# Joining attention and the first dense layer of a three-part kernel into one block

## The chip, the cores and the metric

The kernel runs on one core of a Trainium2 chip. The metric is device time in microseconds (us) of one execution. Five engines of the core matter: TensorE (PE: matmuls and transposes; PEld are its weight loads), VectorE (DVE), ScalarE (ACT), GpSimd (POOL) and SyncE (SP, which here only issues transfers). Each runs its own list of instructions in order, and the lists wait for one another through semaphores.

## The reference

Everything is float32. Attention with a memory term for 4 batches of 8 heads, 576 tokens, 64 columns a head:

```python
scores = where(causal, -1e9, q @ k.T / sqrt(64))
local = softmax(scores) @ v
q_p = where(q > 0, q, exp(q) - 1) + 1
mem_out = (q_p @ M_prev) / (q_p @ z_prev + 1e-6)
x = g * mem_out + (1 - g) * local          # g = sigmoid(beta), heads side by side: 2304 x 512
```

Two dense layers follow:

```python
h = x @ w_in                               # 2304 x 2048
x = (s * maximum(h, 0) ** 2 + b) @ w_out   # 2304 x 512
h = x @ w2_in                              # 2304 x 1024
out = layernorm(h * softmax(h)) * g_ln @ w2_out
```

## The kernel before

There are three parts, each in a Block of its own: attention, the first layer, the second layer. At the end of a Block all engines meet at a barrier. The tensors of a part lie in SBUF and PSUM memory that the next part uses again. What passes from part to part is xT, the tokens turned so that features lie on partitions (4 blocks of 128 features by 2304 tokens), and the small staging buffer of class Stage for raw weights.

**Attention** goes over 32 heads in steps h = -6 to 34; heads come in 16 pairs. Each engine has its own program over the same steps, and at step h the PE works on three heads: scores of head h + 2 (first_rows, second_rows, third_rows, whose row maxima DVE takes from PSUM), the transposed scores of head h (cross, four chunks, of which ACT takes the exponentials in exp_weights and POOL masks the diagonal tiles in mask_weights, L345), and the weighing of the values of head h - 1 (weigh_values, L493, 30 small matmuls, which wait for all masks of that head). After a pair, DVE scales the result (scale_local, L703 to L711), POOL adds the memory half (add_halves, L352, 128x640), the PE turns it (turn_output, L388, five transposes) and ACT copies it into xT (copy_output, L583). The last pair, number 15, does this in steps 32 to 34. The first 512 tokens of xT, all that the first chunk of the layer needs, come from pairs 0 to 3 and are long done by then. SP loads queries, keys and values ahead, and at step 28 the first two blocks of both weight matrices of the layer into the staging buffer (load_win, load_wout).

**The first layer** takes the tokens in five chunks (512, 512, 512, 384, 384), and 16 blocks f of 128 hidden features. A float32 product is made of three rounded ones: a value is cut into a rounded part (hi) and the rest (lo), and hi*hi, lo*hi, hi*lo are summed. For chunk 0, ACT rounds four token blocks (x_hi, L900) and DVE subtracts (x_lo, L903). POOL cuts the weights: for each f first the w_in block (L823 rounds, L826 subtracts, 128x512 each), then the w_out block (L829, L832). The PE then runs hidden(c, f), 12 matmuls into ps_h (L857 to L859), and two blocks later output(c, f), 12 matmuls into ps_y (L872 to L874). Between them stand ACT's relu (L919), DVE's square and scale (L952, L954), ACT's rounding (L925) and DVE's subtraction (L957, g_lo). Inside hidden and output of chunk 0 the waits for weights are

```python
if c == 0:
    pe.wait_ge(win_cut, f + 1)
...
if first:
    pe.wait_ge(wout_cut, f + 1)
pe.wait_ge(g_lo_done, c * FT + f + 1)
```

SP loads w_in block f when block f - 2 is cut (its staging place is then free), and the same for w_out.

**The second layer** goes over 18 tiles of 128 tokens, with a barrier ahead of it in both kernels.

Of the kernel before, what the change touches and what calls it, by code (L numbers as in the profile page):

```python
# [6 lines left out]
F32 = mybir.dt.float32  # L7
# [5 lines left out]
P = 128  # L13
# [14 lines left out]
class Stage:  # L28
# [7 lines left out]
    def __init__(self, nc, ctx, w_in, w_out, v_in, v_out, g_ln):  # L36
        self.w_in, self.w_out, self.v_in, self.v_out, self.g_ln = w_in, w_out, v_in, v_out, g_ln
        self.rows = ctx.enter_context(nc.sbuf_tensor("stage", [P, 4, self.SLOT], F32))
        self.ln_gain = ctx.enter_context(nc.sbuf_tensor("ln_gain", [P, g_ln.shape[0] // P], F32))
# [42 lines left out]
def attention(nc, ctx, xT, q, k, v, M_prev, z_prev, beta, stage):  # L82
# [32 lines left out]
    def sem(name):  # L115
        return ctx.enter_context(nc.semaphore(name))

    q_raw = [sb(f"q_raw{s}", [P, NT, 2, D]) for s in range(2)]
    k_raw = [sb(f"k_raw{s}", [P, NT, 2, D]) for s in range(2)]
    v_raw = [sb(f"v_raw{s}", [P, NT, 2, E1]) for s in range(3)]  # L120
    mz = sb("mz", [P, NPAIR, 2 * E1])
    qT = [sb(f"qT{s}", [P, S]) for s in range(2)]
    cut = [sb(f"cut{s}", [P, 3, S], F32R) for s in range(2)]
    relu_q = [sb(f"relu_q{s}", [P, S]) for s in range(2)]
    fT = [sb(f"fT{s}", [P, W]) for s in range(2)]
    stacked = sb("stacked", [P, 2 * SLOTS, 2, W], F32R)
    Q1, K1 = sb("Q1", [P, SLOTS, 2, W], F32R), sb("K1", [P, LATE, 2, W], F32R)
    least = [sb(f"least{s}", [P, P]) for s in range(2)]
    negT = sb("negT", [P, P])
    pT = [sb(f"pT{s}", [P, NP]) for s in range(2)]  # L130
    spent = sb("spent", [P, sum(keys)])
    rm, rl = sb("rm", [P, NT, 2]), sb("rl", [P, 2, NT])
    t_mem = [sb(f"t_mem{s}", [P, NT, 2, D]) for s in range(3)]
    t_loc = sb("t_loc", [P, NT, 2, D])
    xq = sb("xq", [P, NT, 2 * D])
    mask = sb("mask", [P, FULL * P + P])
    ident = sb("ident", [P, P])
# [46 lines left out]
    STEPS = range(-6, HEADS + 3)  # L184
# [10 lines left out]

    block = ctx.enter_context(nc.Block())
# [17 lines left out]
    @block.sync  # L214
    def _(sp):
# [50 lines left out]
        for h in range(HEADS + 3):  # L266
# [16 lines left out]
    @block.gpsimd  # L283
    def _(pool):
# [70 lines left out]

        for h in STEPS:
            pr = h // 2
            even = h % 2 == 0
            if is_head(h):
                mask_weights(h, 0)  # L360
            if is_head(h + 1):
                if is_head(h):
                    pool.wait_ge(tri_done, h * NT + 2)
                else:
                    pool.wait_ge(phi_done, 1)
                spread_maxima(h + 1)
            if even and is_pair(pr + 2):
                round_queries(pr + 2)
            if is_head(h):
                mask_weights(h, 1)  # L370
            if even and is_pair(pr + 2):
                cut_queries(pr + 2)
            if h == -2:
                clear_keys()
            if not even and is_pair(pr - 1):
                add_halves(pr - 1)
            if is_head(h):
                mask_weights(h, 3)
            if even and is_pair(pr + 1):
                features(pr + 1)  # L380

    @block.tensor
    def _(pe):
# [114 lines left out]

        for h in STEPS:
            pr, even = h // 2, h % 2 == 0  # L500
            ahead, here, behind = is_head(h + 2), is_head(h), is_head(h - 1)
            if ahead or is_head(h + 1):
                first_rows(h + 2)
            if here:
                cross(h, 0)
            if even and is_pair(pr - 2):
                turn_output(pr - 2)
            if h == 0:
                memory(0)
            if not even and is_pair(pr + 3):  # L510
                turn_queries(pr + 3)
            if behind:
                weigh_values(h - 1, (0, 1))
            if ahead:
                second_rows(h + 2)
            if here:
                cross(h, 1)
            if behind:
                weigh_values(h - 1, (2,))
            if even and is_pair(pr + 3):  # L520
                turn_keys(pr + 3)
            if ahead:
                third_rows(h + 2)
            if here:
                cross(h, 2)
            if behind:
                weigh_values(h - 1, (3,))
            if here:
                cross(h, 3)
            if not even and is_pair(pr + 1) and pr + 1 > 0:  # L530
                memory(pr + 1)
            if behind:
                weigh_values(h - 1, (4,))

    @block.scalar
    def _(act):
# [57 lines left out]
        for h in range(-2, HEADS + 3):  # L594
            pr, even = h // 2, h % 2 == 0
            here = is_head(h)
            if here:
                exp_weights(h, 0)
            if even and is_pair(pr - 2):
                copy_output(pr - 2)  # L600
            if not even and is_pair(pr + 3):
                copy_queries(pr + 3)
            if here:
                exp_weights(h, 1)
            if is_pair(pr + 2):
                if even:
                    repeat_queries(pr + 2, 0)
                else:
                    feature_relu(pr + 2)
            if even and is_pair(pr + 3):  # L610
                round_keys(pr + 3)
            if here:
                exp_weights(h, 2)
            if is_pair(pr + 2):
                if even:
                    repeat_queries(pr + 2, 1)
                else:
                    feature_exp(pr + 2)
            if here:
                exp_weights(h, 3)  # L620

    @block.vector
    def _(dve):
# [90 lines left out]

        for h in STEPS:
            pr, even = h // 2, h % 2 == 0
            ahead = is_head(h + 2)
            if ahead or is_head(h + 1):
                first_rows(h + 2)
            if h == 0:  # L720
                scale_memory(0)
            if ahead:
                second_rows(h + 2)
                third_rows(h + 2)
            if even and is_pair(pr + 3):
                cut_keys(pr + 3)
            if h == STEPS[0]:
                dve.memset(words(K1[MINE[1], :, 0, 0:S]), 1.0).then_inc(cleared_dve, 1)
            if h == -3:
                work_out_gates()  # L730
            if not even and is_pair(pr + 1) and pr + 1 > 0:
                scale_memory(pr + 1)
            if even and is_pair(pr - 1):
                scale_local(pr - 1)


def squared_relu_mlp(nc, ctx, xT, w_in, w_out, s, b, stage, win_hi, win_lo):

# [14 lines left out]
    def sem(name):  # L753
        return ctx.enter_context(nc.semaphore(name))
# [3 lines left out]
    wout_hi, wout_lo = (sb(f"wout_{x}", [P, FT, DM], F32R) for x in ("hi", "lo"))  # L758
# [3 lines left out]
    sb_in = sb("sb_in", [P, 2])  # L762
# [4 lines left out]
    w_hi_done = sem("w_hi_done")  # L767
# [26 lines left out]
    block = ctx.enter_context(nc.Block())  # L794

    @block.sync
    def _(sp):
# [20 lines left out]
    @block.gpsimd  # L818
    def _(pool):
        for f in range(FT):  # L820
            pool.wait_ge(win_landed[f % 2], 16 * (f // 2 + 1))
            lanes = slice(f * P, (f + 1) * P)
            pool.tensor_scalar(win_hi[:, :, lanes], win_raw[f % 2], 1.0, 1.0,  # L823
                               ALU.mult, ALU.mult).then_inc(w_hi_done, 1)
            pool.wait_ge(w_hi_done, 2 * f + 1)
            pool.tensor_tensor(win_lo[:, :, lanes], win_raw[f % 2], win_hi[:, :, lanes],  # L826
                               ALU.subtract).then_inc(win_cut, 1)
            pool.wait_ge(wout_landed[f % 2], 16 * (f // 2 + 1))
            pool.tensor_scalar(wout_hi[:, f, :], wout_raw[f % 2], 1.0, 1.0,  # L829
# [7 lines left out]
        for k in range(KT):  # L837
# [5 lines left out]
                               ALU.subtract).then_inc(stage.vin_cut, 1)  # L843

    @block.tensor
    def _(pe):
        def hidden(c, f):

            if c == 0:
# [541 lines left out]
```

## Time and profile before

| what | value |
|---|---|
| time, median of 3 runs | 899.12 us (898.62 to 899.37) |
| the profiled execution: its time, its span | 899.47 us, 897.8 us |
| mean granted TensorE clock | 0.992 of full |
| busy: PE, DVE, ACT, POOL | 858.6, 492.7, 313.9, 259.7 us |
| attention, up to the barrier | 0 to about 269.2 us |
| first layer | about 269.2 to 650 us |

The profile is of one execution. The span runs from its first to its last instruction. Busy time is the time in which an engine works; an engine that is not the bottleneck may idle without cost. A granted clock of 1.00 is TensorE's 2.4 GHz, about 0.5 is 1.2 GHz. Starts of PE rows are exact, while their ends are modelled and overlap the next start; for cadence one reads starts.

### The profile page before, as it was taken

How to read it: one execution, taken by the hardware profiler on the slowest of the kernel's cores; microseconds unless marked ns; L12 is line 12 of the kernel's file. 1: busy time of each engine (PE TensorE's matmuls, PEld its weight loads, DVE VectorE, ACT ScalarE, POOL GpSimd, SP SyncE). 2: the span in 40 equal slices, each digit the busy share in tenths (PEclk: the TensorE clock that was granted, in tenths of full speed). 3: DMA queues.
4: the chain of work that ended last, by engine and by line, in shares of the span. 5: the costliest groups of instructions: out<-in, count | busy, mean ns of one | idle time of the engine just before them, and what ended most of it. 6: DMA issues, size and time to landing. Idle time of an engine off the chain costs nothing. (4 is left out here: it accounts for less than half of the span.)

```text
span 897.8 us, 13246 instructions
## 1 busy us (share of the span) xinstructions
PE 858.6 (96%) x4896; PEld 756.4 (84%) x4896; DVE 492.7 (55%) x1025; ACT 313.9 (35%) x564; POOL 259.7 (29%) x371
## 2 busy tenths in 40 slices
PE   3899999999978999999999999999988999999997
PEld 2799999999876888888888889999986888888886
DVE  6566666666517765433443344444736665566653
ACT  3455556565422222222322222232234223223322
POOL 6366656565539993000000000000600000000000
PEclk9999999999998999999999999999998999999999
DMA  7967575765403432000000000000201000000000
GB/s 169 160 135 162 124 162 123 161 126 123 114 1 95 108 115 60 1 1 1 0 1 1 1 0 1 1 1 1 95 4 44 24 24 23 23 23 23 14 22 36
DMA packets 87511, 51.63 MB, mean 58 GB/s; under 512 B 65184, under 2 KB 73376, under 8 KB 87456
## 3 DMA queue, kind: packets, MB, share of 16 engines
q1 hardware_dynamic: 86112, 50.59, 23.9%
q8 instruction: 35, 0.57, 0.3%
q10 hardware_dynamic: 1344, 0.30, 0.2%
q14 instruction: 20, 0.16, 0.1%
HBM read 27.28 MB, written 4.72 MB: 36 GB/s over the span
## 5 line engine op out<-in xcount | busy, mean ns | idle before, releaser
L952 DVE TENSOR_TENSOR xT<-xT 128x512 f32<-128x512 f32 (+1 forms) x80 | 60.6, 758 | 136.2 <-ACT xT L919 136.1
L857 PE MATMUL ps_h<-x_hi,win_hi 128*128 128x512 f32 (+1 forms) x320 | 118.7, 371 | 5.3 <-POOL win_lo L826 5.3
L858 PE MATMUL ps_h<-x_lo,win_hi 128*128 128x512 f32 (+1 forms) x320 | 118.2, 369 | 0.0
L859 PE MATMUL ps_h<-x_hi,win_lo 128*128 128x512 f32 (+1 forms) x320 | 118.0, 369 | 0.0
L872 PE MATMUL ps_y<-g_hi,wout_hi 128*128 128x512 f32 (+1 forms) x320 | 117.6, 368 | 0.2 <-DVE g_lo L957 0.2
L874 PE MATMUL ps_y<-g_hi,wout_lo 128*128 128x512 f32 (+1 forms) x320 | 117.6, 367 | 0.0
L873 PE MATMUL ps_y<-g_lo,wout_hi 128*128 128x512 f32 (+1 forms) x320 | 117.6, 367 | 0.0
L493 PE MATMUL ps_v<-v_raw,pT 128*128 128x65 f32 (+1 forms) x960 | 107.4, 254 | 1.2 <-DVE t_loc L711 1.2
L493 PEld LDWEIGHTS ps_v<-v_raw,pT 128*128 128x128 f32 (+1 forms) x960 | 101.2, 173 | 6.4 <-issue 4.5
L649 DVE CUSTOM_DVE_ANT_0 spent<-ps_s,mask 128x576 f32<-128x576 f32 (+4 forms) x160 | 81.6, 539 | 44.8 <-PE ps_s L434 44.3
L549 ACT ACTIVATE pT<-ps_x 128x512 f32<-128x512 f32 (+3 forms) x128 | 64.0, 500 | 101.3 <-PE ps_x L478 100.2
L919 ACT ACTIVATE xT<-ps_h 128x512 f32<-128x512 f32 (+1 forms) x80 | 44.3, 553 | 152.4 <-PE ps_h L859 150.6
L925 ACT ACTIVATE g_hi<-xT 128x512 fp32r<-128x512 f32 (+1 forms) x80 | 47.3, 591 | 130.2 <-DVE xT L954 130.2
L957 DVE TENSOR_TENSOR g_lo<-xT,g_hi 128x512 fp32r<-128x512 f32 (+1 forms) x80 | 63.1, 788 | 52.5 <-ACT g_hi L925 52.5
L839 POOL TENSOR_SCALAR win_hi<-stage 128x1024 fp32r<-128x1024 f32 x4 | 4.9, 1228 | 285.2 <-PE ps_h L859 285.2
L1091 POOL TENSOR_TENSOR rstd<-variance,minus_half 128x1 f32<-128x1 f32 x18 | 17.1, 952 | 195.9 <-DVE variance L1302 195.9
L857 PEld LDWEIGHTS ps_h<-x_hi,win_hi 128*128 128x128 f32 x320 | 60.4, 189 | 14.0 <-POOL win_lo L826 6.4
L345 POOL TENSOR_SCALAR_AFFINE_SELECT pT<-pT 128x128 f32<-128x128 f32 (+1 forms) x160 | 42.0, 282 | 95.5 <-ACT pT L549 95.5
L434 PE MATMUL ps_s<-stacked 128*128 128x512 f32 (+2 forms) x192 | 58.8, 390 | 10.8 <-DMA stacked<-cut 6.2
L858 PEld LDWEIGHTS ps_h<-x_lo,win_hi 128*128 128x128 f32 x320 | 60.5, 189 | 7.7
L859 PEld LDWEIGHTS ps_h<-x_hi,win_lo 128*128 128x128 f32 x320 | 60.5, 189 | 7.7
L872 PEld LDWEIGHTS ps_y<-g_hi,wout_hi 128*128 128x128 f32 x320 | 60.1, 188 | 7.9 <-DVE g_lo L957 0.5
(132 smaller groups left out, 1685.5 us busy)
## 6 DMA issues: line engine op xcount, KB each, us to landing
stacked<-cut SPq DMA_DIRECT2D x64, 288.0 KB, 4.9
out<-res SPq DMA_DIRECT2D x18, 256.0 KB, 2.0
k_raw<-in_k SPq DMA_DIRECT2D x32, 128.0 KB, 2.5
v_raw<-in_v SPq DMA_DIRECT2D x32, 128.0 KB, 2.6
stage<-in_moe_w_in SPq DMA_DIRECT2D x16, 256.0 KB, 2.6
stage<-in_moe_w_out SPq DMA_DIRECT2D x16, 256.0 KB, 2.6
q_raw<-in_q SPq DMA_DIRECT2D x30, 128.0 KB, 3.7
stage<-in_moe_w_in SPq DMA_DIRECT2D x4, 512.0 KB, 3.2
```

What stands on the lines that cost most here:

```text
L434: ins = pe.matmul(ps_s[:, S_AT[t] + lo:S_AT[t] + hi], stacked[:, a, 0, P * t:P * (t + 1)], stacked[:, a, 1, lo:hi], start=True, stop=True)
L493: ins = pe.matmul(ps_v[0:m, par, E1 * t:E1 * (t + 1)], pT[par][:, at:at + m], v_raw[h // 2 % 3][:, j, par, :], start=(t == 0), stop=(j == ...
L549: act.activation(pT[h % 2][:, chunk_at[c]:chunk_at[c] + chunk_width[c]], ps_x[:, c % 2, 0:chunk_width[c]], ACT.Exp, scale=SCALE).then_inc( ...
L649: return dve.tensor_tensor_reduce(spent[:, at:at + n], ps_s[:, S_AT[t]:S_AT[t] + n], mask[:, FULL * P + r - n:FULL * P + r], -1.0, HUGE, A ...
L857: pe.matmul(out, win_hi[:, k, w], x_hi[:, k, 0:n], start=(k == 0), stop=False)
L858: pe.matmul(out, win_hi[:, k, w], x_lo[:, k, 0:n], start=False, stop=False)
L859: ins = pe.matmul(out, win_lo[:, k, w], x_hi[:, k, 0:n], start=False, stop=(k == KT - 1))
L872: pe.matmul(out, wout_hi[:, f, w], g_hi[:, r, 0:n], start=(f == 0), stop=False)
L873: pe.matmul(out, wout_hi[:, f, w], g_lo[:, r, 0:n], start=False, stop=False)
L874: ins = pe.matmul(out, wout_lo[:, f, w], g_hi[:, r, 0:n], start=False, stop=(f == FT - 1))
L952: dve.tensor_tensor(r, r, r, ALU.mult).then_inc(square_done, 1)
L957: dve.tensor_tensor(g_lo[:, f % RING, 0:width(c)], r, g_hi[:, f % RING, 0:width(c)], ALU.subtract)\
```

## The change

Attention and the first layer now share one Block, with no barrier between them. Their functions no longer open a Block but return a program for each engine, cut into pieces, and build puts the pieces in order by hand. The order around the seam, each engine for itself (step numbers are those of attention):

- SP: all loads of attention, then s and b (two small ones), then the first two w_in and w_out blocks, then the rest in the order w_in f, w_out f - 2.
- POOL: steps up to 31; cut w_in blocks 0 and 1; steps 32 to 34 (add_halves of pair 15); then w_in 2, w_out 0, w_in 3, w_out 1, and so on.
- PE: steps up to 32 (turn_output of pair 14, weigh_values of head 31); hidden(0, 0); hidden(0, 1); steps 33 and 34 (turn_output of pair 15); hidden(0, 2); output(0, 0); on as before.
- ACT: steps up to 30; step 31 with one x_hi block worked in behind each of the four exponentials of head 31; step 32; relu and rounding of block 0; steps 33 and 34 (copy_output of pair 15); on as before.
- DVE: steps up to 31; the four x_lo blocks; steps 32 to 34 (scale_local of pair 15); on as before.

Where a piece of the layer overwrites memory of attention, a let_go piece waits on semaphores that say that attention is done with it. Tensors of attention are declared in another order, xq, ident and the s and b tensor are moved out of the reused memory, and the cut weights lie block by block (win with hi and lo beside each other, instead of win_hi and win_lo). The second layer reads its weights through second_weights from the same memory. The arithmetic is the same.

```diff
-def attention(nc, ctx, xT, q, k, v, M_prev, z_prev, beta, stage):
+def attention(nc, whole, ctx, xT, xq, ident, q, k, v, M_prev, z_prev, beta):
...
-            if h == HEADS - 4:
-                for f in range(2):
-                    stage.load_win(sp, f)
-                    stage.load_wout(sp, f)
...
+        def let_go():
+            pool.wait_ge(kT_turned, NPAIR)
+            pool.wait_ge(qT_turned, NPAIR)
...
+        def let_go():
+            pe.wait_ge(t_loc_done, NPAIR)
+            pe.wait_ge(xT_done, NPAIR)
...
+        def steps(hs, aside=None):
+            for h in hs:
...
+                if here:
+                    exp_weights(h, 0)
+                    if aside:
+                        aside(0)
...
+        def let_go():
+            act.wait_ge(maxed, 4 * HEADS)
+            act.wait_ge(phi_done, NPAIR)
+            act.wait_ge(mem_done, NPAIR)
+            for p in (NPAIR - 2, NPAIR - 1):
+                stacks_taken(act, p)
...
+def second_weights(win, KT, wide):
+    flat = win[:, :, :, :].rearrange("p f two n -> p (f two n)")
+    return [flat[:, part * KT * wide:(part + 1) * KT * wide].rearrange("p (k n) -> p k n", n=wide)
+            for part in range(2)]
...
+        for f in range(2):
+            stage.load_win(sp, f)
+            stage.load_wout(sp, f)
         for f in range(2, FT):
             sp.wait_ge(win_cut, f - 1)
             stage.load_win(sp, f)
+            if f > 3:
+                sp.wait_ge(wout_cut, f - 3)
+                stage.load_wout(sp, f - 2)
+        for f in (FT - 2, FT - 1):
             sp.wait_ge(wout_cut, f - 1)
             stage.load_wout(sp, f)
...
+        def begin():
+            cut_win(0)
+            cut_win(1)
+
+        def rest():
+            for f in range(2, FT):
+                cut_win(f)
+                cut_wout(f - 2)
+            cut_wout(FT - 2)
+            cut_wout(FT - 1)
...
+        def program(c, aside=None):
             for f in range(FT):
                 hidden(c, f)
+                if aside:
+                    aside(f)
                 if f >= LAG:
-                    output(c, f - LAG, first)
...
+            @block.gpsimd
+            def _(pool):
+                attend, let_go = heads.gpsimd(pool)
+                begin, rest = layer.gpsimd(pool)
+                attend(range(-6, HEADS))
+                let_go()
+                begin()
+                attend(range(HEADS, HEADS + 3))
+                rest()
...
+                def last_output(f):
+                    if f == 1:
+                        attend(range(HEADS + 1, HEADS + 3))
+                    if f == 2:
+                        let_go()
+
+                attend(range(-6, HEADS + 1))
+                program(0, last_output)
+                rest()
...
+                def last_output(f):
+                    if f == 0:
+                        attend(range(HEADS + 1, HEADS + 3))
+
+                attend(range(-2, HEADS - 1))
+                let_go()
+                attend(range(HEADS - 1, HEADS), begin)
+                attend(range(HEADS, HEADS + 1))
+                program(0, last_output)
+                rest()
...
+                attend(range(-6, HEADS))
+                begin()
+                attend(range(HEADS, HEADS + 3))
+                rest()
```

## Rows read from the trace of the kernel before

**Rows 1.** The page, part 1: busy us, share of the span, instructions.

```profile
PE 858.6 (96%) x4896; PEld 756.4 (84%) x4896; DVE 492.7 (55%) x1025; ACT 313.9 (35%) x564; POOL 259.7 (29%) x371
```

**Rows 2.** Waits of PE, 255 to 345 us: total us, times, longest.

```profile
PE ps_h L857 <- POOL win_lo L826: 5.3, 3, 3.5
PE ps_t L388 <- POOL xq L352: 3.0, 1, 3.0
PE ps_v L493 <- DVE t_loc L711: 0.8, 1, 0.8
```

**Rows 3.** Stretches: length, then busy us of each engine, clock, transfers.

```profile
264.50:271.70 7.20, 0.79 (x6) 0.53 (x5) 3.01 (x5) 2.84 (x5) 3.88 (x4) 0.77 0.02 1
271.70:275.30 3.60, 3.52 (x8) 2.81 (x9) 3.27 (x3) 0.00 (x0) 3.52 (x4) 0.51 0.25 73
360.00:500.00 140.00, 140.00 (x619) 115.97 (x618) 55.75 (x87) 36.07 (x61) 0.00 (x0) 1.00 0.00 1
```

**Rows 4.** Waits of PE, 284 to 680 us, after the seam.

```profile
PE ps_hid L1107 <- DVE y_lo L1250: 2.3, 1, 2.3
PE ps_y L872 <- DVE g_lo L957: 0.2, 1, 0.2
```

**Rows 5.** Timeline of PE at the seam: start, us, instruction, count.

```profile
260.86 0.76 PE L388 MATMUL ps_t<-ident,xq 128*128 128x128 f32 x5
261.46 3.07 PE L493 MATMUL ps_v<-v_raw,pT 128*128 128x65 f32 x30
...
271.77 0.79 PE L857 MATMUL ps_h<-x_hi,win_hi 128*128 128x512 f32 x1 [3.50 <-POOL win_lo L826]
...
281.25 0.50 PE L857 MATMUL ps_h<-x_hi,win_hi 128*128 128x512 f32 x1 [1.36 <-POOL win_lo L826]
...
284.10 0.39 PE L872 MATMUL ps_y<-g_hi,wout_hi 128*128 128x512 f32 x1
284.32 0.39 PE L873 MATMUL ps_y<-g_lo,wout_hi 128*128 128x512 f32 x1
```

**Rows 6.** Timeline of ACT: an exponential of head 31, the layer's first relu.

```profile
258.11 0.57 ACT L549 ACTIVATE pT<-ps_x 128x480 f32<-128x480 f32 x1 [1.56 <-PE ps_x L478]
...
276.43 0.60 ACT L919 ACTIVATE xT<-ps_h 128x512 f32<-128x512 f32 x1 [5.00 <-PE ps_h L859]
```

**Rows 7.** Timeline of DVE: last t_loc, the four x_lo, the first g_lo.

```profile
265.02 0.82 DVE L711 TENSOR_TENSOR t_loc<-ps_v,rl 128x640 f32<-128x640 f32 x1
...
269.90 5.07 DVE L903 TENSOR_TENSOR x_lo<-xT,x_hi 128x512 fp32r<-128x512 f32 x4 [4.06 <-ACT x_hi L900]
...
280.07 1.67 DVE L957 TENSOR_TENSOR g_lo<-xT,g_hi 128x512 fp32r<-128x512 f32 x1 [0.70 <-ACT g_hi L925]
```

**Rows 8.** Groups of DVE, 372 to 500 us, with POOL idle: busy, mean ns.

```profile
L903 DVE TENSOR_TENSOR x_lo<-xT,x_hi 128x512 fp32r<-128x512 f32 x4 | 2.5, 686 | 2.8 <-ACT x_hi L900 2.8
```

**Rows 9.** Timeline of POOL: masks and halves, then cuts of weights.

```profile
258.75 0.54 POOL L345 TENSOR_SCALAR_AFFINE_SELECT pT<-pT 128x128 f32<-128x128 f32 x2 [1.65 <-ACT pT L549]
259.25 1.55 POOL L352 TENSOR_TENSOR xq<-t_loc,t_mem 128x640 f32<-128x640 f32 x1
260.75 0.29 POOL L345 TENSOR_SCALAR_AFFINE_SELECT pT<-pT 128x128 f32<-128x128 f32 x1
...
269.27 0.62 POOL L823 TENSOR_SCALAR win_hi<-stage 128x512 fp32r<-128x512 f32 x1 [1.81 <-POOLq L1358]
269.97 1.75 POOL L826 TENSOR_TENSOR win_lo<-stage,win_hi 128x512 fp32r<-128x512 f32 x1
...
279.93 1.26 POOL L826 TENSOR_TENSOR win_lo<-stage,win_hi 128x512 fp32r<-128x512 f32 x1
281.16 1.06 POOL L829 TENSOR_SCALAR wout_hi<-stage 128x512 fp32r<-128x512 f32 x1
```

**Rows 10.** Timeline of SP: the last of the layer's early weight loads.

```profile
236.32 0.51 SPq L66 DMA_DIRECT2D stage<-in_moe_w_out  x1
```

**Rows 11.** The page, part 6: the layer's w_in loads, us to landing.

```profile
stage<-in_moe_w_in SPq DMA_DIRECT2D x16, 256.0 KB, 2.6
```

More of the change, by code:

```diff
@@ L265, in _ @@
         load_values(1)
-        for h in range(HEADS + 3):
+        for h in range(HEADS):
             pr = h // 2
@@ L497, in weigh_values @@
                 ins.then_inc(pv_done, 1)
[L499 to L533, printed above, removed]
@@ L535, in _, with steps @@
-    @block.scalar
-    def _(act):
+        def steps(hs):
+            for h in hs:
+                pr, even = h // 2, h % 2 == 0
+                ahead, here, behind = is_head(h + 2), is_head(h), is_head(h - 1)
+                if ahead or is_head(h + 1):
+                    first_rows(h + 2)
+                if here:
+                    cross(h, 0)
+                if even and is_pair(pr - 2):
+                    turn_output(pr - 2)
+                if h == 0:
+                    memory(0)
+                if not even and is_pair(pr + 3):
+                    turn_queries(pr + 3)
+                if behind:
+                    weigh_values(h - 1, (0, 1))
+                if ahead:
+                    second_rows(h + 2)
+                if here:
+                    cross(h, 1)
+                if behind:
+                    weigh_values(h - 1, (2,))
+                if even and is_pair(pr + 3):
+                    turn_keys(pr + 3)
+                if ahead:
+                    third_rows(h + 2)
+                if here:
+                    cross(h, 2)
+                if behind:
+                    weigh_values(h - 1, (3,))
+                if here:
+                    cross(h, 3)
+                if not even and is_pair(pr + 1) and pr + 1 > 0:
+                    memory(pr + 1)
+                if behind:
+                    weigh_values(h - 1, (4,))
@@ L593, in _ @@
         feature_exp(0)
[L594 to L620, printed above, removed]
@@ L847, in hidden, with tensor @@
+        return begin, rest
+    def tensor(pe):
         def hidden(c, f):
@@ L930, in copy_out, with program @@
                 act.activation(columns(d, c), ps_y[:, d, 0:width(c)], ACT.Copy).then_inc(y_out_act, 1)
[L932 removed]
+        def program(c, aside=None):
             for f in range(FT):
[L934 removed]
+                if f == FT - 1 and c < CHUNKS - 1:
                     cut_chunk(act, c + 1)
@@ L937, in program, with begin, rest, vector @@
                 round_block(c, f)
-                if f == LAG - 1 and behind:
+                if aside:
+                    aside(f)
+                if f == LAG - 1 and c > 0:
                     copy_out(c - 1)
-        cut_chunk(act, 0)
-        for c in range(CHUNKS):
-            program(c, c > 0, c < CHUNKS - 1)
-        copy_out(CHUNKS - 1)
-    @block.vector
-    def _(dve):
+        def begin(k):
+            cut_block(act, 0, k)
+        def rest():
+            for c in range(1, CHUNKS):
+                program(c)
+            copy_out(CHUNKS - 1)
+        return begin, program, rest
+    def vector(dve):
         def square_block(c, f):
@@ L968, in program, with begin, rest, solu_mlp @@
                     dve.wait_ge(sb_landed, 32)
-                if f == FT - 1 and ahead:
+                if f == FT - 1 and c < CHUNKS - 1:
                     cut_chunk(dve, c + 1)
                 square_block(c, f)
-                if f == LAG - 1 and behind:
+                if f == LAG - 1 and c > 0:
                     copy_out(c - 1)
-        cut_chunk(dve, 0)
-        for c in range(CHUNKS):
-            program(c, c > 0, c < CHUNKS - 1)
-        copy_out(CHUNKS - 1)
-def solu_mlp(nc, ctx, yT, w_in, w_out, g_ln, out, stage, win_hi, win_lo):
+        def begin():
+            cut_chunk(dve, 0)
+        def rest():
+            for c in range(CHUNKS):
+                program(c)
+            copy_out(CHUNKS - 1)
+        return begin, rest
+    return Programs(sync, gpsimd, tensor, scalar, vector)
+def solu_mlp(nc, ctx, yT, w_in, w_out, g_ln, out, stage, win):
     DM, FF = w_in.shape
```

327 lines of the change are left out of this document (191 added, 136 removed).

## The prediction

> **What bounds the kernel now.** I read the page's busy times first: PE works 858.6 of 897.8 us [rows 1], so time can be won only where PE stands still or runs slowly. Next come the waits of PE around the seam [rows 2]: 3.0 us for the last pair's sum (turn_output of pair 15, through scale_local and add_halves), and 5.3 us in three pieces for POOL's cut w_in blocks. The third view is the table of stretches [rows 3]. From 264.5 to 271.7 us PE is busy for 0.79 us; in the 3.6 us after that it starts 8 matmuls at a granted clock of 0.51, which is the 1.2 GHz level, while 3.6 us at full clock hold 16 starts (140 us hold 619, that is 0.226 us each). The clock fell after that idle stretch, and a gap that goes takes the slow matmuls with it. The waits after 284 us [rows 4] say that from there to the end of the first layer PE waits 0.2 us in all; the 2.3 us belong to the second layer. So whatever is won or lost before 284.1 us moves everything behind it one for one.
>
> **The most that can be won.** I compare the start of output(0, 0), 284.10 us, with its start in the new order [rows 5]. Between the first value matmul of head 31 (261.46) and 284.10 lie 22.64 us. PE's work in them is 3.0 us of values (3.07 with its modelled end), one turn of 0.6 us (260.86 to 261.46 for the other pair) and three hidden blocks of 12 matmuls. The third, undisturbed one takes 2.85 us from 281.25 to 284.10 with the restart in it, 12 times 0.226 us are 2.71, and I take 2.75. That is 3.0 + 0.6 + 8.25 = 11.85 us, and 22.64 - 11.85 = 10.8 us can go. It is made of 3.0 + 5.3 us of waits, about 1.7 us of half clock (8 starts lost) and some tenths at each of the restarts. The barrier itself has no price of its own here: it lies inside these waits. I use 10.7 us as the ceiling, which puts output(0, 0) at 273.4.
>
> **What the moved work costs, part by part.**
>
> Loads: the first weights are issued by 236.3 us now [rows 10] and stay where they are in SP's queue (no load of attention is behind them); s and b go ahead of them, two issues of some 0.4 to 0.5 us, hidden by over 24 us of slack. The order w_in f, w_out f - 2 issues a load when a place is free, and it lands 2.6 us later [rows 11]; POOL needs w_in 2 some 3 us or more after w_in 0 is cut. Cost 0. The let_go waits are for things that are past by then, cost 0 on POOL and ACT; on PE the let_go waits for copy_output of pair 15, discussed below.
>
> ACT: the four x_hi go into gaps behind the exponentials. The gap ahead of the second was 1.56 us [rows 6], and a block takes 0.6. At most 0.1 us of the later exponentials is delayed. I take 0.
>
> DVE and POOL: here is the price. x_lo takes 0.69 us with POOL idle [rows 8], 1.27 beside POOL's cuts (5.07 for four [rows 7]); the subtraction on POOL takes 1.26 or 1.75, its rounding 0.62 or 1.06 [rows 9]. The rows look like taking turns: g_lo starts at 280.07 and needs 1.67 us, and its end at 281.74 is the end of POOL's subtraction (281.19) plus little more than its own 0.69; POOL's rounding at 281.16 in turn needs 1.06, some 0.44 us of waiting for DVE. The Trainium skill, "SBUF — State Buffer", section "Who interferes with whom", says that a DVE instruction with two SBUF inputs and a GpSimd one that reads SBUF take a shared pair of ports as an exclusive lock, and that one with a single SBUF input is free; by it t_loc, which reads PSUM, costs nothing extra. The trace agrees in these rows, and the rule speaks against this change, because it puts x_lo among POOL's last masks and sums.
>
> First meeting: the second x_hi follows the exponential that starts at 258.11 [rows 6], so the second x_lo is ready at about 258.11 + 0.55 + 0.65 = 259.3 us. POOL starts add_halves of pair 14 at 259.25 [rows 9], and PE needs it at 260.86 with no slack. If POOL goes first, the sum is on time, but x_lo runs ahead of the last mask, which ends at 261.75 or so instead of 261.04, and the values of head 31 start 0.35 us late. If DVE goes first, the sum is late by 0.7 and the mask waits for a third x_lo: 1.0 us late. Were it a sharing of bandwidth instead, 1.55 times 1.75/1.26 makes 0.6 us. It is a near tie; I take 0.7 with 0.35 and 1.0 as bounds.
>
> Second meeting, after the masks: the two cuts, with the remaining x_lo between their instructions. With the mask done at 261.75: x_lo to 262.4, rounding to 263.05, x_lo to 263.7, subtraction to 265.0. PE is through the values at 264.8: 0.2 us of waiting. With the mask at 262.45 the cut ends at 265.05 and PE comes at 265.5: none. The two cases thus meet, near 265.1 to 265.5 for hidden(0, 0), at full clock since PE never stood.
>
> Third: add_halves of pair 15 is now behind w_in 1 in POOL's queue. w_in 1 ends at about 265.0 + 2.1 = 267.1; t_loc, 265.02 + 0.82 now [rows 7], comes at about 266.5, and the sum is ready at 268.7. What waits is turn_output of pair 15, and PE comes to it only after two hidden blocks, 265.3 + 5.5 = 270.8. Hidden by 2.1 us; without those two blocks it would be 3 us of stall, as now. copy_output is done by 272, before output(0, 0).
>
> Fourth: POOL cuts w_in 2 from 268.7. Between two DVE chains a cut takes 1.06 + 0.1 + 1.26 = 2.4 us, up to 2.9 if both instructions wait (1.06 + 0.1 + 1.75 [rows 9]). It ends at 271.1 to 271.6, and PE comes at 270.8 + 0.6 = 271.4: 0 to 0.2 us. w_out 0 ends 2.4 to 3.2 us later, 273.5 to 274.8, and PE comes to output(0, 0) at 274.2. The other thing it needs, g_lo, takes 5.3 us from the start of the relu now (276.43 to 281.74 [rows 6, 7]); the relu is free at 265.3 + 2.9 = 268.2, so g_lo is there at 273.5, 274.3 if one more turn is lost. So 0 to 0.6 us.
>
> Output(0, 0) then starts at 273.9 at best and 274.9 at worst; I take 274.7, nearer to the late end, since each of these waits was at its contended length in the rows. Gain 284.10 - 274.7 = 9.4 us. After that PE takes 2.75 us for a block and POOL 2.4 for a cut, in the order in which PE wants them, so the slack grows by 0.3 each time and the gain stays.
>
> **The sum.** The profiled execution took 899.47 us (span 897.8 and 1.7 around it), 0.35 above the median of 899.12. 899.47 - 9.4 = 890.1 for it, and 889.7 beside the median.
>
> **The rivals.**
> - The meetings are missed or cheap: x_lo falls into POOL's pauses. The gain is 10.2 to 10.8, 888.6 us. For it: POOL's masks leave gaps of over 1 us. Against it: the tie at 259.3.
> - POOL becomes the bound of the first blocks. From the late mask (262.45) with every cut at 2.9: w_in 0 at 265.35, w_in 1 at 268.3, the sum at 270.3, w_in 2 at 273.2, w_out 0 at 276.1. That is a gain of 8.0, and since 2.9 is more than PE's 2.75, each of the next 14 or so pairs of cuts may take 0.3 more: 4 to 8 us of gain, 893.3 us as its middle. For it: POOL works without a pause in this stretch now (3.52 of 3.60 us [rows 3]). Against it: the contended pair of instructions is 2.9 once and 2.4 as a rule.
> - Slower: POOL and DVE keep each other so busy that the cuts of chunk 0 set its pace for all 16 f. It decides when a pair of cuts plus DVE's three instructions needs over 5.5 + 9.4/14 = 6.2 us; now it is 4.9 (twice 2.4), and 6.5 would give about 904 us. Nothing in the rows comes near.
> - The change doesn't do what it says: some wait (a let_go, a load behind a wait in SP's queue) holds the layer until attention is over, as the barrier did. Then the 10.7 us stay, 899 us. Against it: every semaphore waited for is past by the rows' times.
>
> **How the numbers follow.** My forecast 0.56 (gain 8.6 to 10.2: 888.9 to 890.5), cheap meetings 0.22, POOL as bound 0.17, slower 0.03, nothing gained 0.02. The likeliest is 889.7 us. The range runs from the ceiling, 888.3, to a gain of 6.6 us, 892.5, which leaves out half of the third case and the last two. Faster by over 0.2% (1.8 us, about what a measurement of this kernel can tell) 0.95, within it 0.02, slower 0.03.
>
> **What the profile of the changed kernel would show.** PE's waits at the seam shrink from 8.3 to under 2 us; the granted clock stays at 1.00 from 255 to 290; output(0, 0) starts near 274.7; the values of head 31 start 0.3 to 1.0 us later than 261.46; add_halves or the last mask is longer or later than in [rows 9]; the stretch from output(0, 0) to the end of the kernel keeps its length. The prediction is wrong if POOL's cuts hold PE beyond the first output block, if the clock falls at the seam although PE goes on, or if the rest of the kernel changes its length through the moved tensors.

## The result, and the profile after

The changed kernel takes 889.38 us (median of 4 runs, 889.23 to 889.77) against 899.07 us (4 runs) before: ratio 0.9893, 95% interval 0.9876 to 0.9910, 9.7 us faster. The forecast was 889.7 us. The profiled execution took 889.27 us with a span of 887.6 us, 10.2 us less than the one before.

Two views of the changed kernel answer to [rows 3]: the stretches, with the same columns (length, then busy us and number of instructions of PE, PEld, DVE, ACT, POOL; then granted clock, share and GB/s of transfers).

```profile
255.00:264.50 9.50, 8.27 (x72) 7.53 (x72) 5.11 (x7) 4.63 (x9) 6.48 (x10) 1.00 0.01 2
264.50:271.70 7.20, 7.20 (x42) 6.01 (x41) 3.36 (x5) 0.98 (x2) 6.64 (x7) 1.00 0.32 93
271.70:275.30 3.60, 3.60 (x18) 2.94 (x17) 3.26 (x3) 1.28 (x3) 3.52 (x4) 1.00 0.30 107
```

and, from the list of all waits of PE in the execution, those that answer to [rows 2] and [rows 4]:

```profile
...
PE ps_n L1201 <- DVE expo L1388: 3.8, 1, 3.8
...
PE ps_hid L1185 <- DVE y_lo L1328: 2.4, 1, 2.4
...
PE ps_v L498 <- DVE t_loc L739: 1.2, 3, 0.8
...
PE ps_t L393 <- POOL xq L350: 0.5, 1, 0.5
PE ps_y L931 <- DVE g_lo L1028: 0.2, 1, 0.2
```

ps_n and ps_hid belong to the second layer. From 264.5 us on, through the seam, PE is busy all the time at a clock of 1.00, where it was busy 0.79 of 7.20 us before. The 5.3 us of waits for cut w_in blocks are gone, and of the 3.0 us of waiting for a sum 0.5 us is left, now for the sum of pair 14. PE's timeline, answering to [rows 5]:

```profile
261.18 0.77 PE L393 MATMUL ps_t<-ident,xq 128*128 128x128 f32 x5 [0.46 <-POOL xq L350]
261.88 3.17 PE L498 MATMUL ps_v<-v_raw,pT 128*128 128x65 f32 x30
264.98 0.50 PE L916 MATMUL ps_h<-x_hi,win 128*128 128x512 f32 x1
...
270.58 0.71 PE L393 MATMUL ps_t<-ident,xq 128*128 128x128 f32 x5
271.04 0.47 PE L916 MATMUL ps_h<-x_hi,win 128*128 128x512 f32 x1
...
273.89 0.39 PE L931 MATMUL ps_y<-g_hi,wout 128*128 128x512 f32 x1
```

Output(0, 0) starts at 273.89 us instead of 284.10, and from there to the end of the span both kernels take 613.7 us (887.6 - 273.89 and 897.8 - 284.10). So all of the gain lies ahead of that point. To compare kernels I use **the seam**: from the start of the last crossing matmul of head 31 to the start of output(0, 0).

```profile
259.68 0.30 PE L483 MATMUL ps_x<-Q,K 128*128 128x320 f32 x1
```

It takes 273.89 - 259.68 = 14.21 us in the changed kernel. In the kernel before the same matmul starts at 259.89, and the seam is 24.21 us. The gain of the change is 10.0 us; the other 0.2 us of the span lies inside attention, which this execution went through a little faster. Of the 10.0 us, some 7.8 are waits (8.3 us in the rows of PE before, 0.5 now); the other 2.2 are slow matmuls and restarts behind waits, less the little that the first meeting of DVE and POOL costs. DVE and POOL, answering to [rows 7] and [rows 9]:

```profile
259.03 3.34 DVE L965 TENSOR_TENSOR x_lo<-xT,x_hi 128x512 fp32r<-128x512 f32 x3 [1.29 <-ACT x_hi L962]
```

```profile
258.54 0.54 POOL L343 TENSOR_SCALAR_AFFINE_SELECT pT<-pT 128x128 f32<-128x128 f32 x2 [1.50 <-ACT pT L560]
259.05 2.08 POOL L350 TENSOR_TENSOR xq<-t_loc,t_mem 128x640 f32<-128x640 f32 x1
261.07 0.75 POOL L343 TENSOR_SCALAR_AFFINE_SELECT pT<-pT 128x128 f32<-128x128 f32 x1
261.80 1.04 POOL L866 TENSOR_SCALAR win<-stage 128x512 fp32r<-128x512 f32 x1
262.93 1.27 POOL L869 TENSOR_TENSOR win<-stage,win 128x512 fp32r<-128x512 f32 x1
264.16 0.62 POOL L866 TENSOR_SCALAR win<-stage 128x512 fp32r<-128x512 f32 x1
264.86 1.28 POOL L869 TENSOR_TENSOR win<-stage,win 128x512 fp32r<-128x512 f32 x1
266.45 1.57 POOL L350 TENSOR_TENSOR xq<-t_loc,t_mem 128x640 f32<-128x640 f32 x1 [0.31 <-DVE t_loc L739]
267.99 0.62 POOL L866 TENSOR_SCALAR win<-stage 128x512 fp32r<-128x512 f32 x1
268.69 1.29 POOL L869 TENSOR_TENSOR win<-stage,win 128x512 fp32r<-128x512 f32 x1
```

The second x_lo starts 0.02 us ahead of add_halves of pair 14, and the sum takes 2.08 us instead of 1.55; the last mask takes 0.75 instead of 0.29. The last x_lo still holds the first rounding of w_in 0 up (1.04 us). From there to the subtraction of w_in 2 POOL works at 0.62 and 1.28 us an instruction.

### The profile page after: what moved, and what is told of

Its sections match the earlier page's. It is cut to its first block and busy times, and to the rows that moved or that the text cites. A ratio compares the mean times of both kernels' runs of the same rounds, so it can differ in the third digit from the quotient of the medians.

```text
span 887.6 us, 13240 instructions
## 1 busy us (share of the span) xinstructions
PE 856.8 (97%) x4896; PEld 755.3 (85%) x4896; DVE 491.8 (55%) x1025; ACT 313.3 (35%) x564; POOL 259.9 (29%) x371
## 5 line engine op out<-in xcount | busy, mean ns | idle before, releaser
L931 PE MATMUL ps_y<-g_hi,wout 128*128 128x512 f32 (+1 forms) x320 | 117.5, 367 | 0.2 <-DVE g_lo L1028 0.2
L916 PE MATMUL ps_h<-x_hi,win 128*128 128x512 f32 (+1 forms) x320 | 117.7, 368 | 0.0
L918 PE MATMUL ps_h<-x_hi,win 128*128 128x512 f32 (+1 forms) x320 | 117.5, 367 | 0.0
L933 PE MATMUL ps_y<-g_hi,wout 128*128 128x512 f32 (+1 forms) x320 | 117.5, 367 | 0.0
L932 PE MATMUL ps_y<-g_lo,wout 128*128 128x512 f32 (+1 forms) x320 | 117.5, 367 | 0.0
L917 PE MATMUL ps_h<-x_lo,win 128*128 128x512 f32 (+1 forms) x320 | 117.5, 367 | 0.0
L897 POOL TENSOR_SCALAR win<-stage 128x1024 fp32r<-128x1024 f32 x4 | 4.9, 1230 | 280.8 <-PE ps_h L918 280.8
L931 PEld LDWEIGHTS ps_y<-g_hi,wout 128*128 128x128 f32 x320 | 60.0, 188 | 7.9 <-DVE g_lo L1028 0.5
L916 PEld LDWEIGHTS ps_h<-x_hi,win 128*128 128x128 f32 x320 | 60.1, 188 | 7.7
L932 PEld LDWEIGHTS ps_y<-g_lo,wout 128*128 128x128 f32 x320 | 60.1, 188 | 7.5
L917 PEld LDWEIGHTS ps_h<-x_lo,win 128*128 128x128 f32 x320 | 60.1, 188 | 7.6
```

The lines of the kernel that those rows point to most:

```text
L916: pe.matmul(out, hi, x_hi[:, k, 0:n], start=(k == 0), stop=False)
L917: pe.matmul(out, hi, x_lo[:, k, 0:n], start=False, stop=False)
L918: ins = pe.matmul(out, lo, x_hi[:, k, 0:n], start=False, stop=(k == KT - 1))
L931: pe.matmul(out, wout[:, f, HI, w], g_hi[:, r, 0:n], start=(f == 0), stop=False)
L932: pe.matmul(out, wout[:, f, HI, w], g_lo[:, r, 0:n], start=False, stop=False)
L933: ins = pe.matmul(out, wout[:, f, LO, w], g_hi[:, r, 0:n], start=False, stop=(f == FT - 1))
```

## The experiments

All are edits of the changed kernel. The time is a median with the ratio to the kernel before on the same chip; that kernel's median was 899.07, 899.33, 900.01 and 899.20 us on the four chips, so ratios and not medians compare across them. The seam is that of one profiled execution.

In these executions the part behind the seam is 612.0 to 614.9 us long. The first layer has no share in that: from output(0, 0) to the first layer's last matmul it takes 386.5 to 386.7 us in all of them (in the kernel before it thus ends at 670.6 us, not at about 650, as the table of its profile has it). The rest goes with the clock at the start of the second layer: where the granted clock of 640 to 700 us is 0.91, the part behind the seam is 614.7 to 614.9 us; at 0.94 it is 613.1 to 613.7; at 0.97, in one, 612.0. Attention ahead of the seam varies too: its last crossing matmul starts between 258.8 and 260.2 us. So times of two kernels 1 us apart are not told apart, while the seam repeats where PE does not stand (14.21 us in both executions of the changed kernel that were profiled). Kernels with a gap at the seam were profiled once each, and their seams hold a price of the clock that, as shown below, is not the same for the same gap.

| kernel | seam us | median us | ratio to before |
|---|---|---|---|
| before | 24.21 | 899.07 | 1 |
| changed | 14.21 | 889.38 | 0.9893 (0.9876 to 0.9910) |
| changed, again | 14.21 | 889.20 | 0.9874 (0.9857 to 0.9890) |
| old order in one block | 22.03 | 898.06 | 0.9984 (0.9974 to 0.9994) |
| the same, old order of cuts too | 22.08 | 897.36 | 0.9981 (0.9972 to 0.9991) |
| weights early alone | 22.86 | 896.64 | 0.9969 (0.9953 to 0.9985) |
| tokens early alone | 20.97 | 895.77 | 0.9965 (0.9953 to 0.9978) |
| last turn first | 19.25 | 893.32 | 0.9934 (0.9917 to 0.9950) |
| last sum first | 21.52 | 897.58 | 0.9980 (0.9969 to 0.9992) |
| last sum first, gap filled | 19.24 | 893.22 | 0.9932 (0.9916 to 0.9949) |
| tokens late | 18.39 | 894.19 | 0.9948 (0.9931 to 0.9964) |
| tokens a head earlier | 13.64 | 889.06 | 0.9881 (0.9864 to 0.9897) |
| x_lo made twice | 14.58 | 890.02 | 0.9888 (0.9871 to 0.9904) |
| w_out cut first | 15.62 | 889.19 | 0.9886 (0.9870 to 0.9903) |

My theory is that the gain comes from the order at the seam, by which PE always has work while DVE, ACT and POOL finish the last pair and prepare the layer. The rivals are the barrier itself, POOL's cuts as the bound, and the price of x_lo among the heads.

### The barrier alone: the old order in one block

```diff
 # POOL
-                attend(range(-6, HEADS))
+                attend(range(-6, HEADS + 3))
                 let_go()
                 begin()
-                attend(range(HEADS, HEADS + 3))
                 rest()
 # PE
-                attend(range(-6, HEADS + 1))
-                program(0, last_output)
+                attend(range(-6, HEADS + 3))
+                let_go()
+                program(0)
 # ACT and DVE: all steps of attention first, too
```

> One block and no barrier, but every engine finishes attention before it begins the layer, as before the change. If the gain comes from the order at the seam (my theory), PE stands again while the last pair is summed and turned, x_lo and the first cut begin after it, and the clock falls: output(0, 0) starts at about 280 us (273.9 in the changed kernel, 284.1 before) and the time is 895 to 896.5 us. What is better than before is one w_out cut that no longer stands ahead of w_in 1, and the barrier's tenths. If the barrier itself was what cost (rival), the time is 891 us or less.

The seam is 22.03 us, 2.2 less than before. That is a smaller gain than I expected, with output(0, 0) at 281.91 instead of about 280 and a median of 898.06 instead of 895 to 896.5 us, but it is far from the rival's 891 us. The rows of PE:

```profile
267.50 0.76 PE L393 MATMUL ps_t<-ident,xq 128*128 128x128 f32 x5 [2.98 <-POOL xq L350]
270.64 0.77 PE L916 MATMUL ps_h<-x_hi,win 128*128 128x512 f32 x1 [2.38 <-DVE x_lo L965]
281.91 0.47 PE L931 MATMUL ps_y<-g_hi,wout 128*128 128x512 f32 x1 [0.32 <-DVE g_lo L1028]
```

The wait of 2.98 us for the sum is back in full, hidden(0, 0) waits for x_lo, and the clock falls:

```profile
271.70:275.30 3.60, 3.60 (x9) 2.18 (x8) 3.19 (x3) 0.00 (x0) 3.17 (x3) 0.50 0.25 73
```

To see what of the 2.2 us is the order of the cuts, a second kernel also cuts and loads w_in f, w_out f in turn.

```diff
         def begin():
-            cut_win(0)
-            cut_win(1)
+            pass
 
         def rest():
-            for f in range(2, FT):
+            for f in range(FT):
                 cut_win(f)
-                cut_wout(f - 2)
-            cut_wout(FT - 2)
-            cut_wout(FT - 1)
+                cut_wout(f)
```

> The kernel with the old order in one block, and POOL also cuts in the old order w_in f, w_out f. What is left against the kernel before is the barrier and where the tensors lie. My theory: x_lo still holds hidden(0, 0) at about 270.6, 1.1 us earlier than before, since POOL starts to cut at 267.4 instead of 269.3; w_in 2 comes later than with the new order; the stretch is 22.0 to 22.8 us. If the order of the cuts gave those 2.2 us, it is 24.

The seam is 22.08 us, the same within 0.1: with the rest in the old order, the order of the cuts gives nothing that shows. Leaving out the barrier (with the tensors moved, which was not tried apart) gives 2.1 us. Hidden(0, 0) starts 10.8 instead of 11.9 us after the last crossing matmul, and POOL, which begins to cut right behind its sum, keeps PE waiting 0.4 us for the next blocks instead of 1.8. The other 7.8 us are the order, with the clock that it keeps up.

### One part undone

Last turn first: PE turns pair 15 before it begins the layer.

```diff
                 def last_output(f):
-                    if f == 1:
-                        attend(range(HEADS + 1, HEADS + 3))
...
-                attend(range(-6, HEADS + 1))
+                attend(range(-6, HEADS + 3))
                 program(0, last_output)
```

> The changed kernel, but PE turns the last pair's output before hidden(0, 0) instead of behind hidden(0, 1). My theory: POOL's sum is ready at about 268.0 us and PE is free at 265.0, so it stands 3.0 us, and output(0, 0) starts at 276.9 us: 892.4 us, or 894 if the clock falls in that gap. A rival, that POOL's cuts would have held PE anyway, says under 1 us more than the changed kernel: 889.4 to 890.4.

PE waits 2.98 us, as said, and the clock falls too. The time is 893.32 us and the seam is 5.0 us longer: 3.0 of waiting and 2.0 of slow matmuls and a g_lo that is 0.35 us late. The two hidden blocks ahead of the turn are what hides the last pair's sum.

Last sum first means that POOL's steps 32 to 34 stand ahead of its first cuts (the edit of POOL above, alone).

> The changed kernel, but POOL adds the last pair's halves before it cuts w_in 0 and 1. My theory: the sum ends at 267.6 us or so, w_in 0 is cut at 269.6, PE stands some 4.7 us and then runs at half clock for a while: output(0, 0) starts between 278.6 and 280.3, time 894 to 895.8 us. If early cuts are worth little (rival: x_lo is what holds PE), less than 2 us over the changed kernel.

```profile
270.07 0.79 PE L916 MATMUL ps_h<-x_hi,win 128*128 128x512 f32 x1 [4.91 <-POOL win L869]
```

The wait is 4.9 us as expected, but output(0, 0) comes at 281.31, a microsecond later than the latest that I gave: the seam is 7.3 us longer, of which 2.4 are not waiting. The time is 897.58 us instead of 894 to 895.8.

Tokens late means x_hi after step 32 and x_lo after the last scale_local.

> The changed kernel, but x_hi is made after step 32 and x_lo after the last scale_local. My theory: the sum of pair 14 is on time again and the values of head 31 start 0.6 us earlier, but the fourth x_lo comes at about 269.6 us because each takes 1.1 to 1.3 beside POOL; hidden(0, 0) ends at 270.3 instead of 267.9, and the time is about 891.9 us (+2.5). If x_lo among the heads costs more than it gives (the rule against the change), the time is 889 or less.

The time is 894.19 us instead of 891.9, the seam 18.39 us. The values of head 31 do start 0.63 us earlier (1.57 us behind the last crossing matmul, against 2.20), so the meeting was what delayed them. But PE waits 2.1 and 0.9 us for x_lo and then runs slowly for some matmuls, which I had not counted. The rule that speaks against the change sees a real price and is outweighed by far.

### The clock measured apart: the gap filled

To the kernel with the last sum first, 20 surplus matmuls are added where PE waits.

```diff
+        def fill():
+            pe.wait_ge(x_hi_done, KT)
+            for _ in range(20):
+                pe.matmul(ps_h[:, RING - 1, 0:512], x_hi[:, 0, 0:P], x_hi[:, 0, 0:512], start=True, stop=True)
...
+                fill()
                 program(0, last_output)
```

> The kernel that sums first, with 20 surplus matmuls of 128x512 on PE (into a PSUM bank that is overwritten later) in the 4.9 us in which PE waits for w_in 0. My theory: 2.3 us of that kernel's loss is the clock, which fell in the gap. With PE busy it stays at 1.00, hidden(0, 0) starts at 270.1 as without the filling, and output(0, 0) follows 8.9 us later instead of 11.2; the time is 2.3 us shorter. If the slow start has another cause (weights or g_lo late), the 11.2 us stay.

The same stretch in the kernel with the last sum first,

```profile
271.70:275.30 3.60, 3.60 (x11) 2.79 (x10) 0.00 (x0) 0.00 (x0) 2.75 (x4) 0.52 0.37 109
```

and in this one:

```profile
271.70:275.30 3.60, 3.60 (x18) 2.93 (x18) 1.58 (x2) 0.60 (x1) 2.95 (x4) 1.00 0.27 77
```

```profile
264.52 4.84 PE L957 MATMUL ps_h<-x_hi 128*128 128x512 f32 x20
269.57 0.50 PE L916 MATMUL ps_h<-x_hi,win 128*128 128x512 f32 x1 [0.21 <-POOL win L869]
```

From hidden(0, 0) to output(0, 0) it takes 8.89 us (269.57 to 278.46), against 11.24 (270.07 to 281.31) with the gap empty, and 8.91 in the changed kernel. The seam is 2.28 us shorter, although the layer starts no earlier. The clock's share of this idle gap is shown, from one execution of each kernel: 2.3 us. The medians differ by 4.4 us. In the two profiled executions, whose spans differ by 4.3 us, 1.5 us of that lies behind the seam and 0.6 us in attention, where the two kernels are the same.

### One part alone

Weights early alone has POOL as in the changed kernel and PE, ACT and DVE in the old order.

> One block, POOL cuts w_in 0 and 1 ahead of the last sum as in the changed kernel, but tokens and PE keep the old order (attention first). If the parts of the change are worth something only together (my theory), x_lo holds PE as in the kernel with the old order, hidden(0, 0) starts near 270.6 us, and the stretch from the last crossing matmul to output(0, 0) is 21.5 to 22.0 us, against 22.0 with the old order, 24.2 before and 14.2 after the change; time 897 to 898. If each part has its own price that adds up, the early cuts, whose undoing cost 7.3 us, give several us here: under 20 us.

Tokens early alone has ACT and DVE prepare the tokens early, while POOL and PE keep the old order. PE's new order alone was not tried.

> One block, x_hi and x_lo early as in the changed kernel, but POOL sums before it cuts, and PE turns the last output before the layer. My theory: the cut of w_in 0 ends at 270.0 and holds PE, the same start as in the kernel that only sums first, less the turn that is already done: 20.7 to 21.0 us for that stretch, time about 896.5. If parts add up (undoing the early tokens cost 4.2 us): 18 us or less.

The seams are 22.86 and 20.97 us, against 22.03 with neither: the early weights alone lose 0.8 us in the seam, the early tokens alone gain 1.1. The loss is more than expected; the turn of pair 15 shows a part of it, slow already:

```profile
266.77 1.33 PE L393 MATMUL ps_t<-ident,xq 128*128 128x128 f32 x5 [2.98 <-POOL xq L350]
```

The clock had fallen before these five transposes, where they took 0.76 us in the kernel with the old order. Copy_output ends 0.6 us later by it, and x_hi and x_lo follow it; then the first x_lo took turns with a POOL that had more to cut, and hidden(0, 0) lost another 0.8 us. With the tokens early alone the transposes were slow too, and hidden(0, 0) waited for something that the expectation does not name:

```profile
267.81 1.33 PE L393 MATMUL ps_t<-ident,xq 128*128 128x128 f32 x5 [2.98 <-POOL xq L350]
269.93 0.77 PE L916 MATMUL ps_h<-x_hi,win 128*128 128x512 f32 x1 [0.80 <-ACT xT L594]
```

This is the let_go of PE, which waits for copy_output of pair 15. The copy ended at 269.82 us and the cut of w_in 0 at 269.68, so the 20.97 us are as expected but in part by luck: two waits ended nearly together. Since the slow transposes cost some 0.6 us in these two kernels and nothing in the one with the old order, the two seams are known to about that much. That neither part gives several microseconds alone stands all the same.

Both early together with PE in the old order is the kernel with the last turn first, 19.25. Undone one by one, the three parts cost 5.0, 7.3 and 4.2 us, 16.5 together, where they are worth 7.8: PE waits for whichever of sum, weights and tokens comes last, so each is worth little until the others are there.

### The meeting of DVE and POOL

In the kernel with the tokens a head earlier x_hi stands behind the exponentials of head 30, so that x_lo runs in one go.

```diff
-                attend(range(-2, HEADS - 1))
+                attend(range(-2, HEADS - 2))
                 let_go()
-                attend(range(HEADS - 1, HEADS), begin)
-                attend(range(HEADS, HEADS + 1))
+                attend(range(HEADS - 2, HEADS - 1), begin)
+                attend(range(HEADS - 1, HEADS + 1))
```

> The changed kernel, but the four x_hi stand behind the exponentials of head 30 instead of head 31, so that x_lo runs in one go after t_loc of pair 14, from 256.3 to 259.1 us, and is through when add_halves of pair 14 starts. My theory: add_halves takes 1.55 us again instead of 2.08, the last mask 0.29 instead of 0.75, the values of head 31 start 0.4 to 0.6 us earlier, 888.8 to 889.0 us. If the delay of the values is not from this meeting, the same time as the changed kernel.

DVE and POOL of this kernel:

```profile
256.14 2.62 DVE L965 TENSOR_TENSOR x_lo<-xT,x_hi 128x512 fp32r<-128x512 f32 x4
```

```profile
256.30 1.31 POOL L343 TENSOR_SCALAR_AFFINE_SELECT pT<-pT 128x128 f32<-128x128 f32 x2 [1.29 <-ACT pT L560]
258.44 0.71 POOL L343 TENSOR_SCALAR_AFFINE_SELECT pT<-pT 128x128 f32<-128x128 f32 x2 [0.83 <-ACT pT L560]
259.13 1.54 POOL L350 TENSOR_TENSOR xq<-t_loc,t_mem 128x640 f32<-128x640 f32 x1
260.63 0.28 POOL L343 TENSOR_SCALAR_AFFINE_SELECT pT<-pT 128x128 f32<-128x128 f32 x1
```

The sum takes 1.54 us and the last mask 0.28 again; in exchange two masks of head 31 wait, of which only 0.2 us reach PE. The seam is 13.64 us, 0.57 shorter and the shortest of all. The time, 889.06 against 889.20 us for the changed kernel on the same chip, doesn't resolve it.

In the kernel with x_lo made twice DVE makes each block of chunk 0 two times, one after the other.

```diff
+            if c == 0:
+                eng.tensor_tensor(x_lo[:, k, 0:width(c)], columns(k, c), x_hi[:, k, 0:width(c)],
+                                  ALU.subtract).then_inc(x_lo_once, 1)
+                eng.wait_ge(x_lo_once, k + 1)
             eng.tensor_tensor(x_lo[:, k, 0:width(c)], columns(k, c), x_hi[:, k, 0:width(c)],
```

> The changed kernel, but DVE makes each x_lo block twice (the first of the two is surplus work). If DVE and POOL take turns instruction by instruction (the lock), add_halves of pair 14 still waits for one x_lo only, 2.1 us, the mask stays near 0.75, and the two cuts behind them wait a turn each: w_in 0 at 264.7 to 265.3 instead of 264.2, and the time stays within 0.3 us of the changed kernel's. If they share bandwidth, add_halves and the mask grow with the doubled work, and the values of head 31 start over 0.5 us later.

POOL and then DVE of this kernel:

```profile
258.71 2.08 POOL L350 TENSOR_TENSOR xq<-t_loc,t_mem 128x640 f32<-128x640 f32 x1
260.74 0.75 POOL L343 TENSOR_SCALAR_AFFINE_SELECT pT<-pT 128x128 f32<-128x128 f32 x1
```

```profile
258.70 0.69 DVE L967 TENSOR_TENSOR x_lo<-xT,x_hi 128x512 fp32r<-128x512 f32 x1 [0.56 <-ACT x_hi L963]
259.42 1.92 DVE L970 TENSOR_TENSOR x_lo<-xT,x_hi 128x512 fp32r<-128x512 f32 x1
```

With twice the work on DVE, the sum takes 2.08 us and the mask 0.75, to the hundredth what they took before: each POOL instruction waits for the one DVE instruction in progress, and no more. The next x_lo in turn takes 1.92 us, about the rest of the sum and its own 0.69. This is taking turns, not sharing. The Trainium skill, "SBUF — State Buffer", section "Who interferes with whom", adds that the order of issue decides who blocks; the trace agrees, since x_lo, issued 0.01 us ahead of the sum, went through in 0.69. What doubling did cost, 0.37 us of seam, is w_in 2, cut later because POOL now waited for a turn in several instructions. The time, 890.02 us, is 0.8 above the changed kernel's instead of within 0.3, with 614.8 us behind the seam in the profiled execution.

### The order of the cuts

In the kernel with w_out cut first, from w_out 0 on, cut_wout(f - 2) stands ahead of cut_win(f).

> The changed kernel, but from w_out 0 on POOL cuts w_out f - 2 ahead of w_in f. If the order of the cuts matters at the start (my theory), w_in 2 comes one cut later, 272.4 instead of 270.0 us, PE wants it at 271.04, and the time is 1.4 us more, 890.8 us. If POOL has a whole cut of slack there (rival), no change.

PE's wait, in its timeline:

```profile
271.56 0.50 PE L916 MATMUL ps_h<-x_hi,win 128*128 128x512 f32 x1 [1.18 <-POOL win L869]
```

The seam is 15.62 us, 1.4 longer, as expected: there is less than one cut of slack at hidden(0, 2). The time, 889.19 us instead of 890.8, doesn't show it. In the profiled execution attention ahead of the seam was 1.0 us shorter (258.80 us to the last crossing matmul, against 259.83 in the changed kernel's second profile) and the part behind it 0.4 us (613.2 against 613.6), which hides the 1.4 us. So the price of this order is shown by the trace alone. The changed kernel, run again as the measure:

> The changed kernel once more, as the measure for the other three on the same chip: 889.4 us.

Its median is 889.20 us (887.19 to 889.73), its seam 14.21 us.

## Why the prediction was right

- **Where the time is**: right. Behind output(0, 0) both kernels take 613.7 us, and the seam holds the 10.0 us.
- **The ceiling, 10.7 us**: right. The kernel with the tokens a head earlier, which meets POOL least, is 24.21 - 13.64 = 10.6 us under the kernel before. The part of the clock, taken at 1.7 us, was right for the kernel before. As a general price it is too low: with the last sum first it was 2.3, and this is a part of why I put the kernels with an idle gap too early.
- **The first meeting, 0.7 us**: right in kind and size. DVE went first, and the values of head 31 started 0.63 us later (2.20 us after the last crossing matmul, instead of 1.57). One of its readings is not: g_lo ended at 281.74, 0.55 us after POOL's subtraction (281.19), which is less than its own 0.69 and not "little more". And the rule, as the prediction words it, says too much. t_loc did take the same 0.82 us beside a subtraction of POOL, but DVE's scaling (L954), which also has one SBUF tensor as its input, takes 1.40 us beside POOL's cuts and 0.55 with POOL idle.
- **Meetings two to four, 0.6 us** (1.3 us from the ceiling's 273.4 to 274.7, less 0.7 for the first meeting): the term that was mis-sized. PE waited 0 us for them. w_in 0 was cut at 264.20, before PE was free at 264.98; w_in 2 at 269.98, where PE came at 271.04; w_out 0 and g_lo at 272.4 and 273.0, where PE came at 273.89. I gave POOL the contended 2.4 us for each cut. The cut of w_in 0 took that (its rounding met the last x_lo), but between the last x_lo and the first relu DVE has nothing to do save scale_local, and w_in 1 and w_in 2 took 2.0 each. That puts output(0, 0) at 273.9 instead of 274.7, or 0.6 us early when the 0.2 us of attention are taken out.
- **Cover for the last pair**: right. Its sum ended at 268.0, its turn came at 270.6, and without the two hidden blocks PE stood the 3.0 us.
- **Rivals**: POOL as the bound did not appear; the barrier alone is worth 2.1 us, with the tensors moved, where the prediction gave it no price of its own; waits for loads or let_go did not appear on PE. What the prediction did not say is that its parts are of much use only together.
- **The size**: 9.4 us forecast, 9.7 measured, 10.0 in the seam. That the medians differ by only 0.3 us from the forecast is in part luck, since a median of this kernel is good to about 1 us; the seam, 0.6 us better than forecast, is the fairer measure.

## What to carry to other kernels

Where one stage ends and the next begins, list what the busiest engine needs next (here a sum, weights, tokens) with the time of each: only when the last of them is covered does most of the time come back, so try such a change whole. Hide the tail of the old stage behind blocks of the new one (two here; the sum was ready at 268.0 us and the first block ended at 267.9, so one may nearly do, which was not tried), and order each helper engine by what the busy engine wants first. Compare such kernels by one stretch of the trace, start to start, when the noise of the time is as large as the step.

## What the runs showed of the hardware

- The cost of a fallen clock does not follow from the gap alone. After 7 us with hardly any work the kernel before made 8 slow starts of matmuls of 512 columns (about 0.43 us each); after 4.9 us of waiting the kernel with the last sum first made 11, and after 3.0 us that with the last turn first made 8 or 9. Six kernels have the same gap of 2.98 us ahead of five transposes. These took 0.76 or 0.77 us in three of them, 0.93 in the one with the old cuts, and 1.33 in the two with one part early. With the weights early alone the granted clock was down to 0.50 before the gap ended (266.5 us); with the old order it was still 1.00 through the transposes and fell behind them, near 268.7. What sets the moment was not tried.
- The same shows where the second layer starts, behind its barrier. With the same work, the part behind output(0, 0) took 612.0 to 614.9 us in the profiled executions, and its length goes with the granted clock between 640 and 700 us: 0.97 in the shortest, 0.91 in the five longest, 0.94 in the others.
- DVE and POOL take turns to the hundredth of a microsecond: 2.08 and 0.75 us for the same two POOL instructions, whether DVE makes each x_lo once or twice beside them.
